# Order of the low halves and of the transposed-row copies in an MLP block

## The reference

```
attention:  phi(x) = [exp(p - max|p|), exp(-(p - max|p|))],  p = x @ w_phi
            out = phi(q) (phi(k)^T v) / (phi(q) . sum phi(k) + 1e-6)
MLP:        h = x @ w_in ;  g = h * clip(h + 3, 0, 6) / 6 ;  y = g @ w_out
experts:    e = argmax(y @ w_gate) ;  out = gate * sigmoid(y @ w_ogate)[e] * relu(y @ w1[e]) @ w2[e]
```

## Time and profile before

| what | value |
|---|---|
| median of three runs | 881.70 us |
| the profiled execution | 881.79 us |
| its span | 880.1 us |
| PE busy | 842.0 us (96%) |
| DVE busy | 572.0 us (65%) |
| ACT busy | 413.4 us (47%) |
| POOL busy | 180.2 us (20%) |
| L845, H on PE | 1152 matmuls, 200.9 us busy |
| L856, O on PE | 864 matmuls, 280.4 us busy in two groups |
| mean granted clock of PE | 0.993 |

### The profile page before, as it was taken

One profiled execution on the slowest core, in us unless ns is written; L12 is line 12 of the kernel. 1 busy time (PEld: TensorE's weight loads), 2 busy tenths in 40 slices (PEclk: granted clock), 3 DMA queues, 4 the chain that ended last, 5 costly groups with the idle time before them and its releaser, 6 DMA issues.

```text
span 880.1 us, 19939 instructions
## 1 busy us (share of the span) xinstructions
PE 842.0 (96%) x7258; PEld 562.5 (64%) x7259; DVE 572.0 (65%) x1200; ACT 413.4 (47%) x838; POOL 180.2 (20%) x208
## 2 busy tenths in 40 slices
PE   6999999999999999999999999999999999999994
PEld 5888788786555455455555455455777767777763
DVE  4777788886887897897897887863652444222221
ACT  5666578766556656566566566542310111111110
POOL 4444367652000001001001001001121222111100
PEclk9999999999999999999999999999999999999998
DMA  7345664543463563555555556256345762656610
GB/s 221 103 164 176 199 180 161 176 137 108 173 236 148 192 216 144 203 216 183 193 191 228 191 191 228 96 206 239 124 160 187 276 224 72 236 202 222 232 53 13
DMA packets 44885, 156.13 MB, mean 177 GB/s; under 512 B 7895, under 2 KB 12247, under 8 KB 38161
## 3 DMA queue, kind: packets, MB, share of 16 engines
q1 hardware_dynamic: 38896, 138.33, 44.2%
q0 software_dynamic: 5760, 16.80, 5.5%
q10 hardware_dynamic: 160, 0.07, 0.0%
HBM read 109.44 MB, written 47.47 MB: 178 GB/s over the span
## 4 chain that ended last, share of the span: by engine, by line
PE 70%; DVE 13%; issue 6%; ACT 5%; DMA 3%; POOL 2%; ACTq 0%; DVEq 0%; POOLq 0%
PE ps L856 15%; PE ps L845 13%; PE ps L952 12%; PE ps L940 12%; PE ps L761 4%; PE ps L706 3%; PE ps L733 3%; DVE u_mx L1443 2%; DVE relu L1526 2%; DVE arena L1231 2%; DMA arena<-split 2%; ACT arena L1054 2%; ACT arena L1159 1%; DVE arena L1470 1%; POOL arena L530 1%
## 5 line engine op out<-in xcount | busy, mean ns | idle before, releaser
L845 PE MATMUL ps<-arena,w_in_sb 128*128 128x384 f16 x1152 | 200.9, 326 | 1.3 <-issue 1.3
L856 PE MATMUL ps<-w_out_sb,arena 128*128 128x512 f16 x576 | 171.3, 379 | 5.2 <-DVE stage L1531 4.8
L845 PEld LDWEIGHTS ps<-arena,w_in_sb 128*128 128x128 f16 x1152 | 110.8, 98 | 75.1 <-issue 1.8
L1208 ACT ACTIVATE x_sb<-ps 128x512 f16<-128x512 f32 x54 | 31.6, 596 | 203.2 <-PE ps L940 177.9
L940 PE MATMUL ps<-x_sb,arena 128*128 128x128 f16 x2112 | 122.0, 219 | 4.3 <-issue 3.1
L940 PEld LDWEIGHTS ps<-x_sb,arena 128*128 128x128 f16 x2112 | 119.4, 98 | 8.5 <-issue 5.0
L952 PE MATMUL ps<-arena,x_sb 128*128 128x512 f16 x528 | 117.9, 379 | 0.0
L856 PE MATMUL ps<-w_out_sb,stage 128*128 128x512 f16 x288 | 109.1, 379 | 0.0
L1054 ACT ACTIVATE arena<-ps,arena 128x128 f32<-128x128 f32 x288 | 79.4, 382 | 55.2 <-DVE arena L1233 52.0
L1177 ACT ACTIVATE arena<-relu 128x384 f16<-128x384 f32 x96 | 50.2, 523 | 116.9 <-DVE relu L1526 115.6
L856 PEld LDWEIGHTS ps<-w_out_sb,arena 128*128 128x128 f16 x576 | 55.1, 98 | 65.5 <-issue 9.7
(11 more groups left out here) (211 smaller groups left out, 999.3 us busy)
## 6 DMA issues: line engine op xcount, KB each, us to landing
arena<-split SPq DMA_DIRECT2D x36, 1024.0 KB, 6.0
arena<-in_moe_w SPq DMA_DIRECT2D x16, 2048.0 KB, 13.4
split<-arena SPq DMA_DIRECT2D x16, 2048.0 KB, 7.4
arena<-in_qkt SPq DMA_DIRECT2D x15, 576.0 KB, 6.4
stage<-in_moe_w_in SPq DMA_DIRECT2D x16, 512.0 KB, 4.2
stage<-in_moe_w_out SPq DMA_DIRECT2D x16, 512.0 KB, 5.4
x_sb<-rows POOLq DMA_DIRECT2D x27, 257.0 KB, 3.0
arena<-in_v SPq DMA_DIRECT2D x32, 128.0 KB, 4.4
```

Source lines behind the costliest of these rows:

```text
L845: last = nc.tensor.matmul(ps[:, HB[f % GB], 0:BN], w_in_sb[:, lw, c, f * P:(f + 1) * P], xt[:, a, c, lx, :], start=c == 0 and lw + lx == 0 ...
L856: last = nc.tensor.matmul(ps[:, YB + r, :], g_sb[lg_][:, f % GB, r * P:(r + 1) * P], w_out_sb[:, lw, f, :], start=f == 0 and lg_ + lw == 0 ...
```

## The change

Two edits. The set of steps in which DVE makes the low half straight behind the product grows from 0, 1, 15 to 0, 1, 2, 3, 15. And ACT's copy of transposed rows stands one step sooner (step 4 + c, in block 5 step 3 + c) and in front of the unit's high halves instead of behind them. PE's order is as it was, and no instruction is added or taken away.

```diff
+SOON = (0, 1, 2, 3, FC - 1)
@@ scalar, mlp_block
                     if post and f == 0:
                         rows_hi(n - 1)
+                    if post and Y_AT + 1 <= f + ahead // 2 < Y_AT + 1 + DC:
+                        copy_yt(n - 1, f + ahead // 2 - Y_AT - 1, XB)
                     k, j = divmod(f - UNIT_AT, 5)
                     if 0 <= k < units and j == 3:
                         unit_hi(n * 3 + k, (odd + k) % 2, 0)
                     if 0 <= k < units and j == 4:
                         unit_hi(n * 3 + k, (odd + k) % 2, 2)
-                    if post and Y_AT + 2 <= f + ahead // 2 < Y_AT + 2 + DC:
-                        copy_yt(n - 1, f + ahead // 2 - Y_AT - 2, XB)
@@ vector, mlp_block
                     gate_chunk(n, f)
-                    if f in (0, 1, FC - 1):
+                    if f in SOON:
                         gate_lo(n, f)
...
-                    if f not in (0, 1, FC - 1):
+                    if f not in SOON:
                         gate_lo(n, f)
```

## The result

The changed kernel takes 890.65 us (median of 4 runs, 890.39 to 893.41) against 882.16 us before on the same chip (4 runs). The ratio is 1.0103, with a 95% interval of 1.0079 to 1.0126: 1% slower. The forecast was 890.2. By the medians the change costs 8.5 us, by the ratio 9.1.

What follows compares the result with a forecast made beforehand. PE was taken as the bound, its O and T waits 9.2 us together. Four longer blocks (+10.20), block 0 (-0.45) and block 5 (-1.24) sum to +8.5 on a median of 881.70: 890.2 us, range 885 to 893.

Steps and rivals of the forecast that it cites:

- O(2) and T(1) stop waiting: PE in blocks 1 to 4: waits of 1.28 us at O(2) and 1.10 at T(1) go, 2.38 a block.
- the 1.14 from product to low half: On DVE, from a product's start to a low half straight behind it: 0.55 plus 0.59 idle, 1.14 us.
- The scale is 1.8 late: Step 4: the unit's scale comes 1.8 us later through DVE's idling, so O(4) loses 0.31, O(5) 1.21, O(6) 0.25.
- the bound: Scale's delay at its lower end, 1.37 us: copy 0 holds the high halves anyway; O(4) loses nothing, O(5) 1.48.
- Copy 3 is the dearest spot: Step 7: copy 3 waits on ACT for T(3), delaying x_hi, relu 8 and low half 8; O(8) loses 0.83 us.
- A block is 2.55 longer: Blocks 1 to 4: new waits 4.93 us less old ones 2.38, so 2.55 each, +10.2 for four.
- Block 3's gap hides as much as before: The 1.28 us issue gap at the loop's second pass hides as much new wait as old, so block 3 changes alike.
- Blocks 0 and 5: Block 0 loses its O(2) wait, -0.45 us; block 5, with one unit and no x_hi, nets -1.24.
- rival 1: DVE's two waits are free, leaving 2.06 us a block: +6.5, 888.2 us; chance 0.06.
- rival 2: Copy 3 finds T(3) done and DVE catches up in steps 6 to 10: faster, 877.6 us; chance 0.06.
- Rival 3: Both old waits go and slack of later low halves swallows the rest: -11.3, 870.4 us; chance 0.04.
- rival 4: Copy 3 doesn't wait but DVE doesn't catch up: +0.9 a block, +2 in all, 883.7 us; chance 0.08.

Runs made afterwards that it cites:

- the first experiment: Only low halves 2 and 3 moved straight behind their product, copies left as before, against the kernel before the change: 896.37 us, ratio 1.0148.

## Why the prediction was right

- **O(2) and T(1) stop waiting.** Right; so is the 1.14 from product to low half (284.70 to 285.84).
- **The scale is 1.8 late.** Right in effect, wrong in size: u_all comes 0.72 us behind u_red, not 1.01; 0.14 of the difference is POOL's reduction, which took 0.35 us against 0.49 before. The high halves were held by copy 0 anyway (293.67, high halves from 294.34), as the bound said. O(4) therefore shows no wait (0.31 forecast), and O(5) is at 300.69, which is the worked-out 301.14 less the 0.45 of block 0. Measured by starts, O(4) loses 0.08 and O(5) 1.44: the 1.52 that the forecast had split as 0.31 and 1.21.
- **Copy 3 is the dearest spot.** Right. With 0.45 taken off, T(3), O(8), O(10) and the last transpose were expected at 307.11, 314.12, 323.60 and 340.02, and are at 307.11, 314.13, 323.59 and 340.01. The lost time by starts is 0.84, 0.78, 0.23 at O(12) and 1.21, against 0.83, 0.79, 0.23 and 1.21. The share of copy 3 was argued in the forecast; that the copy, by its step, is the cause is shown by putting it back (0.9998).
- **A block is 2.55 longer.** It was 2.77 in block 1 and 2.46 in block 4. The term that is missing: H(0) of the next block follows the fourth copy of the next rows, which now ends at 344.43 (start 343.65, 0.78 long). H(0) starts at 344.56 where 344.34 was worked out. It counts once and not in every block, because in block 4 both ends are late by it.
- **Block 3's gap hides as much as before.** Wrong for the profiled execution: the gap was 1.95 us instead of 1.28 and the slow clock added 1.7 to H(0) to H(2). O(5) waits 0.90 there instead of 1.27, so it hid 0.4 us where before it hid the 1.28 at O(2). The profiled execution is therefore 3 us above the forecast's sum, and the median agrees with the sum to half a microsecond. What the other executions did at that place isn't known, so part of this close agreement may be luck.
- **Blocks 0 and 5.** -0.46 and -1.42 against -0.45 and -1.24.
- **Rivals.** The two waits of DVE are not free (rival 1): with the copies in front, adding them turns -4.7 into +2.6 us, and low half 2 alone moves the wait to O(3). The rows keep 0.59 us idle in front of each. The Trainium skill, "VectorE: DVE Perf Modes", The DRAIN you can't avoid, says that a semaphore between chained Vector instructions costs nothing extra. No run here tests this for a wait on the own engine; here the wait is on ACT, so the sentence doesn't bear on it, and rival 1 isn't what it says. Catching up (rival 2) failed at copy 3, which waits 1.60 us; its other half, that DVE catches up behind step 6, holds for O(8) to O(12) once copy 3 is put back. Rival 3 is out by O(5), which waits 1.27, and rival 4 by copy 3.

## What to carry to other kernels

When an instruction waits in an in-order queue, count what stands behind it, not only who asked for it: here one copy moved one step sooner found its input not made, and putting it back gained 9.3 us, as much as the two kinds of wait that were to be removed (9.2). To bring a dependent step forward without idle time, put an independent piece of about the handoff's length in between, as half a search pair for 1.1 us did; look then where the next wait appears, because most of the gain can go there. Two edits that each aim at a visible wait are worth trying apart, since one of them in another form (the copies in front, in their old steps) was a gain.

## What the hardware showed that was not expected

Where T(1) waited for 2.75 to 3.81 us (the first experiment, five blocks), the granted clock went to 0.50 each time, for about 3.4 us in four blocks and 6.8 in one: in two blocks before T(1) began, in the others during T(1) or early in the H behind it. The H behind it took 1.0 to 1.9 us longer than 2.11. No other kernel shows this in that place; with both low halves early and the copies in front, T(1) waited 1.63 and H kept its length.

At the loop's second pass PE stood 1.28 us before, 1.34 with the low halves alone, and 1.81 to 2.20 in the ten other kernels. Behind it H(0) to H(2) took 7.70 us at a granted clock down to 0.50 in five of these ten (waits of 1.95, 2.06, 2.07, 2.12 and 2.20) and 6.02 at full clock in the other five (1.81, 1.96, 2.02, 2.07, 2.11). The length of that gap alone doesn't decide it; what does stays open, and so does why the gap is longer there. It is worth about 1.7 us in an execution.
